# Logits ahead of the second carried set in a linear-attention step, with two waits of the scores taken out

## The reference, cut to what matters

```python
for t in range(S):
    kt, vt, rt = (k[:, :, t], v[:, :, t], r[:, :, t])
    cur = np.einsum('bhd,bhe->bhde', u[None] * kt, vt)
    y[:, :, t] = np.einsum('bhd,bhde->bhe', rt, state + cur)
    state = w[None, :, :, None] * state + np.einsum('bhd,bhe->bhde', kt, vt)
...
x = attn_out.transpose(0, 2, 1, 3).reshape(B * S, H * D)
logits = x @ phi            # 3072 x 384 by 384 x 32
```

## Time and profile before

| | us |
|---|---|
| median of 3 runs | 278.39 |
| lowest and highest run | 277.0, 281.28 |
| profiled execution, own time | 277.07 |
| its span, first to last instruction | 275.2 |
| TensorE busy | 258.7 (94%) |
| VectorE busy | 154.7 (56%) |

### The profile page before, as it was taken

The page is one execution under the profiler, slowest core; times in us unless marked ns, Lnnn a source line. Parts: engine busy times, 40 slices in busy tenths (PEclk is TensorE's granted clock), DMA queues, the critical chain, the costliest instruction groups (busy, mean ns, idle before and its releaser), DMA issues.

```text
span 275.2 us, 10447 instructions
## 1 busy us (share of the span) xinstructions
PE 258.7 (94%) x4505; PEld 218.1 (79%) x4505; DVE 154.7 (56%) x320; ACT 89.3 (32%) x175; POOL 30.5 (11%) x45
## 2 busy tenths in 40 slices
PE   8789899999999998999998799999999999999992
PEld 8768687888787884433477599999999999999991
DVE  5787798889898874435032594532523534435313
ACT  1224445545545543031230552222222222222200
POOL 3222122222212215000000000000000000000000
PEclk9999999999999999999999779999999999999999
DMA  5975899999999999999507500030110300300203
GB/s 155 340 241 171 290 319 387 392 390 378 403 403 407 330 416 417 424 355 427 230 2 265 197 0 0 0 115 0 53 61 0 114 0 0 114 0 16 101 0 120
DMA packets 16324, 55.30 MB, mean 201 GB/s; under 512 B 1936, under 2 KB 5200, under 8 KB 15408
## 3 DMA queue, kind: packets, MB, share of 16 engines
q1 hardware_dynamic: 13216, 43.90, 43.1%
q10 hardware_dynamic: 3088, 11.14, 10.5%
HBM read 50.32 MB, written 4.72 MB: 200 GB/s over the span
## 4 chain that ended last, share of the span: by engine, by line
PE 86%; DMA 4%; DVE 3%; issue 2%; SPq 1%; ACT 1%; POOL 0%; ACTq 0%; DVEq 0%; POOLq 0%
PE ps L1189 12%; PE ps L1188 12%; PE ps L1190 12%; PE ps L922 8%; PE ps L945 6%; PE ps L960 6%; PE ps L969 5%; PE ps L934 4%; PE ps L1173 4%; PE ps L1060 4%; PE ps L1082 4%; PE ps L974 3%; DMA ind<-dmaj 2%; DMA wraw<-wb 2%; PE ps L1029 2%
## 5 line engine op out<-in xcount | busy, mean ns | idle before, releaser
L823 DVE SCALAR_TENSOR_TENSOR hl<-ps,hh 128x512 fp32r<-128x512 f32 x48 | 33.0, 690 | 58.7 <-ACT hh L568 58.7
L1189 PE MATMUL ps<-w2l,hh 128*128 128x384 f32 x192 | 65.3, 340 | 0.0
L1188 PE MATMUL ps<-w2h,hh 128*128 128x384 f32 x192 | 65.1, 339 | 0.0
L1190 PE MATMUL ps<-w2h,hl 128*128 128x384 f32 x192 | 65.0, 338 | 0.0
L568 ACT ACTIVATE hh<-ps 128x512 fp32r<-128x512 f32 x48 | 28.7, 600 | 75.8 <-PE ps L1173 75.8
L1189 PEld LDWEIGHTS ps<-w2l,hh 128*128 128x128 f32 x192 | 36.6, 191 | 1.7
L1188 PEld LDWEIGHTS ps<-w2h,hh 128*128 128x128 f32 x192 | 36.6, 191 | 0.7
L1190 PEld LDWEIGHTS ps<-w2h,hl 128*128 128x128 f32 x192 | 36.6, 191 | 0.0
L435 POOL TENSOR_TENSOR kt<-intk,kttab 128x384 f32<-128x384 f32 x24 | 24.2, 1009 | 71.0 <-DVE rkb L638 62.8
L638 DVE TENSOR_TENSOR rkb<-ind,tab 128x1024 f32<-128x1024 f32 x24 | 29.9, 1247 | 1.4 <-DMA ind<-dmaj 1.4
L922 PE MATMUL ps<-rkb 64*64 64x128 f32 x768 | 27.3, 273 | 0.0
(11 more groups left out here) (163 smaller groups left out, 295.9 us busy)
## 6 DMA issues: line engine op xcount, KB each, us to landing
ind<-dmaj SPq DMA_DIRECT2D x22, 512.0 KB, 8.1
wearly<-wa ACTq DMA_DIRECT2D x21, 512.0 KB, 7.1
intk<-tmaj SPq DMA_DIRECT2D x24, 384.0 KB, 6.9
wearly<-wa SPq DMA_DIRECT2D x4, 1536.0 KB, 11.3
out<-acc SPq DMA_DIRECT2D x5, 768.0 KB, 3.6
wlate<-wa SPq DMA_DIRECT2D x4, 768.0 KB, 9.3
wlate<-wa SPq DMA_DIRECT2D x2, 1536.0 KB, 11.5
wmid<-wa SPq DMA_DIRECT2D x1, 1536.0 KB, 8.4
```

Of the source, the lines that this page charges most:

```text
L823: v.scalar_tensor_tensor(out=hl[:, f % 4, :], in0=ps[:, f % 4, :], scalar=0.0, in1=hh[:, f % 4, :].bitcast(F32), op0=ALU.max, op1=ALU.subt ...
L1188: mm(o, a_h, w2h[:, f, :], start=(f == 0), stop=False)
L1189: mm(o, a_h, w2l[:, f, :], start=False, stop=False)
L1190: ins = mm(o, a_l, w2h[:, f, :], start=False, stop=(f == KF - 1))
```

## The change

`logits` is called between `turn` and the second carried set, with its wait for `lts_ready` in the step ip == 1; the wait for `in_done` and the second carried set come behind it. `scores` waits for `ur_ready` alone. All lines below L914 have one number less in the new kernel.

```diff
             def scores(n, ip):
-                pe.wait_ge(pre_ready, n + 1)
+
                 pe.wait_ge(ur_ready, n + 1)
-                pe.wait_ge(att_ready, n + 1)
                 go()
...
                 carried(ip, True)
                 turn(n)
+                if ip == 1:
+                    pe.wait_ge(lts_ready, c + 1)
+                logits((ip - 1) % PAIRS)
                 pe.wait_ge(in_done, n + 1)
                 go()
                 carried(ip, False)
-                if ip == 1:
-                    pe.wait_ge(lts_ready, c + 1)
-                logits((ip - 1) % PAIRS)
                 within(n, ip)
```

## The result

| | before | after |
|---|---|---|
| median, us (20 runs each) | 278.45 | 281.77 |
| lowest to highest, us | 276.63 to 281.28 | 278.52 to 284.77 |
| ratio | | 1.0122 (95%: 1.0093 to 1.0151) |
| profiled execution, own time, us | 277.07 | 278.52 |
| its span, us | 275.2 | 276.7 |

The changed kernel is slower by 1.2%, 3.4 us. The forecast was 281.0 us, with 1.0 to 1.4% slower.

A forecast was written before the change was run, and what follows sets the result against it. Bound: the 3.59 us chain from sta through increments, scores, mask product and copies. Steps of 3.85 add 3.4 us, the first four steps 0.1: + 3.5, giving 280.6 (profiled) or 281.9 (median), stated as 281.0; range 277.4 to 284.0 us.

The forecast's parts named there:

- the chain sta, increments, scores, mask product, copies: In each recurrence step, from one sta to the next: 0.53 + 1.60 + 0.05 + 1.41 = 3.59 us, the bound before the change.
- The seams: TensorE pauses at tile shape changes: two per step instead of three, transposes to logits 0.53, logits to carried set 0.36 us.
- the second rival: Same mechanism, lower price: short pause between transposes and logits (0.45) or sooner VectorE start; 278.6 us, chance 18%.
- The cost of the late signal: Second carried set ends 1.34 us behind the transposes, sta starts at 1.48 instead of 1.19, 0.29 later.
- The removed waits: The scores' waits for att_ready and pre_ready never held anything; removal put at nothing, at most 0.3 us in all.
- The new step 3.85: Recurrence step after the change: 1.97 + 0.40 + 1.48 = 3.85 us, against 3.59.
- the second chain: Through VectorE's queue: sta, scaling, stb, first carried set, transposes, back to sta; 3.56 us before the change.
- The branch gives part of the loss back: Each loop's 4.00 us branch step has TensorE idle 0.41; increments 0.58 behind sta are covered, making a loop 15.40.
- The fourth rival: Slower than 2%: nothing given back at branches and in the first steps, 24 x 0.28 = 6.7 us, 283.8; chance 16%.
- The sum, + 3.5: Whole recurrence: 3.4 us counted step by step after the first four steps, plus 0.1 in those four.
- The sign that would have been against me: The stage behind the recurrence changing its length by more than 0.5 us would show the prediction wrong.

The follow-up runs named there:

- the kernel without logits: The kernel before, with the logits deleted from the 24 steps; ratio 1.0056, median 280.32 us.
- short scaling: A quarter of VectorE's scaling given to GpSimd: on the changed kernel, ratio to before 1.0062, median 280.54 us; on the kernel before, ratio 1.0018.
- logits between the sets: The kernel before, with logits between the two carried sets in the transposes' place and transposes where the logits stood; ratio 1.0054, median 280.37 us.
- the late signal alone: The kernel before, matmul order kept, with the semaphore releasing sta set by the logits' last matmul; ratio 1.0162, median 283.46 us.
- the first experiment: The kernel before, with only the two waits of the scores taken out; ratio 0.9981, median 277.57 us.
- the logits first: Logits ahead of the transposes, both between the two carried sets, in the other order than in the change; ratio 1.0149, median 283.25 us.

## Why the prediction was right, point by point

- **What bounds the kernel: the chain sta, increments, scores, mask product, copies, 3.59 us.** Right. Less work on TensorE (the kernel without logits) or on VectorE (short scaling) and an earlier signal (logits between the sets) all leave a full loop at 14.7 to 14.9, but for one of 15.97 with a low clock. That all three parts of the chain are needed I read from the rows; no run shortened the chain itself.
- **The seams.** Transposes to logits 0.54 (forecast 0.53), logits to carried set 0.36 (0.36). The short pause of the second rival doesn't exist. The products with v start 1.11 behind the transposes (1.13). That is worth little, as stated: at most the 0.05 us a loop by which the shortest loop with the late signal alone is the longer one. The Trainium skill's rule on drains (TensorEngine Tiling (Array Packing), Key Properties) agrees with the seams; the drain that is saved by it isn't on the chain.
- **The cost of the late signal.** Its end + 1.34 and `sta` + 1.48, both as forecast; 0.14 between them, which I had from one place in the first step only. That place was less clean than I took it for: VectorE wasn't free there, since its scaling before that `stb` is on record from 11.05 to 12.95 and `stb` starts at 12.93. The 0.14 came true in each of steps 4 to 23. The run with the late signal alone shows that this is the cause.
- **The removed waits: nothing.** Right by the first experiment.
- **The new step 3.85.** Measured 3.86, and the second chain (VectorE's queue) is the one that holds it inside a loop, by the run with the short scaling.
- **The branch gives part of the loss back.** Right in kind, a little off in size. I had the increments start 0.58 behind `sta` there and be covered. The weight loads of the changed kernel show:

```profile
60.35 0.63 PEld L959 LDWEIGHTS ps<-pt,intk 64*48 64x48 f32 x32
61.40 0.52 PEld L933 LDWEIGHTS ps<-intk,kt 64*64 64x64 f32 x30 [0.42 <-issue]
```

  and VectorE beside them:

```profile
60.72 0.41 DVE L660 SCALAR_TENSOR_TENSOR sta<-stb,pw,ps 128x192 f32<-128x192 f32 x1 [0.17 <-PE ps L944]
61.05 1.22 DVE L638 TENSOR_TENSOR rkb<-ind,tab 128x1024 f32<-128x1024 f32 x1
62.19 0.41 DVE L660 SCALAR_TENSOR_TENSOR stb<-sta,pw,ps 128x192 f32<-128x192 f32 x1
```

  Increments start 61.40 - 60.72 = 0.68 behind `sta`. The products with v are 0.1 longer in their loads (0.63 for 0.52), as their first half now waits for the first copy and their second for the second one: in the loops' steps the first load starts 0.11 to 0.14 behind the end of the first copy and the seventeenth 0.12 behind that of the second, 0.12 us after the sixteenth (inside a loop 0.04 before the change). From these increments to the transposes at 63.14 it is 1.74 and from there to the next `sta`, at 64.61, 1.47: with the 0.68 that is 3.89, 0.04 more than I gave the chain through VectorE's queue. So this one step isn't covered, as I had said it was: the step behind a branch takes 66.08 - 62.19 = 3.89 in place of 3.85, and a loop 15.47 to 15.50 in place of 15.40. The fourth rival, with nothing given back at the branches (15.9 a loop), didn't come about.
- **The sum, + 3.5.** The 20 runs give + 3.4 (0.0122 x 278.45). In the two profiles the recurrence ends 4.15 later: 3.74 from the `stb` of step 4 to the last `sta`, where I had 3.4, and 0.41 in the first four steps, where I had 0.1 (`stb` of step 4 at 31.20 against 30.79). So that the total agrees to 0.1 us is luck in part. That start isn't settled by two traces, for it varies with the execution: with the two waits alone the fifth step's `stb` starts at 29.73, with the logits first at 33.20. How much of the + 3.4 lies there stays open.
- **The sign that would have been against me: the stage behind the recurrence longer or shorter by more than 0.5 us.** The soft experts take 42 us in both traces. The stage after them is 2.5 us shorter, by its low stretch, which I had not foreseen; it doesn't bear on the chains.

## What to carry to other kernels

Ask of each semaphore what it releases and how late it may be, before a group of instructions is moved ahead of its setter: here 0.36 us of logits moved in front of a signal that had 0.07 us to spare inside a loop (0.21 from its last pass to `sta`, less 0.14), and the loss was what lay beyond that. Where two chains lie within a few hundredths of each other, as 3.59 and 3.56 here, an engine at 98% can be relieved of 5% of its busy time with hardly a gain (0.07 us a loop), and nearly all of a further delay counts. A saved seam or drain is worth something only on the chain that holds the step.

## What the runs showed of the hardware

- VectorE's `sta` started 0.14 us behind the end of the matmul that it waits for (68.34 to 68.48), and the mask product 0.05 us (64.73 to 64.78). The number of semaphores alone doesn't decide it: `stb` waits for two in the code, from step 4 on, and with the short scaling on the changed kernel, where it always waits for TensorE, it starts 0.05 to 0.06 us behind the last increment. What differs in the traces is that the wait for `car_done` is an instruction of its own ahead of `sta` (at 68.41 in this step), while the mask product and `stb` carry TensorE's semaphore themselves. That this is the reason wasn't tested.
- The start of the program is less steady than its loops. The fifth step's `stb` started between 29.73 and 33.20 us in ten traces, with idle times of TensorE put down to issue at varying places. In three of the ten the granted clock also fell to its low level near there, in the fourth or fifth slice (of 7 us), and one step's increments and scores took 2.0 to 2.7 us in place of 1.6; two of these have the latest starts (32.80 with the late signal alone, 33.20 with the logits first), and the third has the loop of 15.97 us (logits between the sets):

```profile
PEclk9997999999999999999999869999999999999998
...
PEclk9999799999999999999995799999999999999998
```

  The first is the kernel with the logits first, the second the one with the logits between the sets. The fourth of the late starts (32.61, short scaling on before) has no low slice, so the clock isn't all of it. Apart from that one loop, the full loops of a trace lie within 0.2 us of each other.
- The low clock fell near the start of the chosen expert in nine of the ten profiled executions and not in the one of the changed kernel; between the two profiles of before and after it goes with 2.5 us. The whole of this change is 3.4 us, so comparing two profiled executions by their spans would have shown less than half of it.
